# The group norms of the opening moved behind the masks of levels 1 and 2, and fewer warm matmuls in the turn

## The reference, cut to what matters

```python
# delta-rule attention: batch 4, heads 8, sequence 768, head size 48
k_n = k / (norm(k) + 1e-6)
for t in range(768):
    y[t] = q[t] @ state
    state += beta[t] * outer(k_n[t], v[t] - state^T k_n[t])
# gated layer: 3072 tokens, 384 -> 1536 -> 384
x = (sigmoid(x @ w_gate) * (x @ w_val)) @ w_out
# routed layer: 8 experts, one per token, 384 -> 1024 -> 384
e = argmax(cosine(x, expert_emb) / tau);  gate = softmax probability of e
out = gate * (relu(x @ w1[e]) @ w2[e])
```

## Time and profile before

| | |
|---|---|
| median of 3 executions | 1217.78 us (1216.74 to 1219.96) |
| the profiled execution | 1220.51 us, its span 1218.8 us |
| TensorE busy | 1191.5 us, 98% of the span |
| VectorE, ScalarE, GpSimd busy | 57%, 41%, 48% |
| mean granted clock of TensorE | 0.995 of 2.4 GHz |
| chain that ended last | TensorE 91%, VectorE 3%, transfers 2% |

### The profile page before, as it was taken

How to read it: one execution, slowest core, us unless ns; L and a number is a source line. 1 busy time by engine, 2 the same in 40 slices (tenths; PEclk the granted TensorE clock), 3 DMA queues, 4 the chain that set the end, 5 groups by cost and what they waited for, 6 DMA issues and landing times.

```text
span 1218.8 us, 29243 instructions
## 1 busy us (share of the span) xinstructions
PE 1191.5 (98%) x11548; PEld 1090.4 (89%) x11548; DVE 696.1 (57%) x1539; ACT 498.6 (41%) x1143; POOL 579.4 (48%) x590
## 2 busy tenths in 40 slices
PE   6899999999999999999999999999999999999997
PEld 2669999999999999999999999999968899989996
DVE  5665566766566666656666665653564945555000
ACT  5644433343443334344433434442214444444443
POOL 5773334333343434324343432322337877777764
PEclk9999999999999999999999999999989999999999
DMA  7451011001111111110111111002016431443110
GB/s 225 113 170 29 24 40 30 30 30 30 36 29 36 30 30 29 30 43 24 34 30 32 27 30 36 8 22 88 31 34 234 140 127 57 156 165 107 45 39 1
DMA packets 48247, 74.76 MB, mean 61 GB/s; under 512 B 7797, under 2 KB 36789, under 8 KB 48116
## 3 DMA queue, kind: packets, MB, share of 16 engines
q1 hardware_dynamic: 41396, 61.82, 15.7%
q0 software_dynamic: 6720, 11.07, 3.0%
HBM read 61.59 MB, written 12.65 MB: 61 GB/s over the span
## 4 chain that ended last, share of the span: by engine, by line
PE 91%; DVE 3%; DMA 2%; ACT 1%; issue 1%; POOL 1%; SPq 1%; POOLq 0%; DVEq 0%
PE ps L1330 27%; PE ps L1345 13%; PE ps L1569 6%; PE ps L1585 6%; PE ps L1195 3%; PE ps L1574 3%; PE ps L1290 3%; PE ps L1589 3%; PE ps L1299 3%; PE ps L1220 3%; PE ps L1212 3%; PE ps L1223 2%; PE ps L1350 2%; PE ps L1599 2%; PE ps L1297 2%; PE ps L1267 2%
## 5 line engine op out<-in xcount | busy, mean ns | idle before, releaser
L440 POOL TENSOR_TENSOR gl<-sg,gh 128x256 fp32r<-128x256 f32 x144 | 108.2, 751 | 392.1 <-ACT gh L994 392.0
L1330 PE MATMUL ps<-xh,wgh 128*128 128x256 f32 x864 | 263.7, 305 | 0.0
L1330 PE MATMUL ps<-xl,wgh 128*128 128x256 f32 x864 | 243.4, 282 | 0.0
L1330 PE MATMUL ps<-xh,wgl 128*128 128x256 f32 x864 | 242.7, 281 | 0.0
L664 DVE TENSOR_TENSOR MP<-ps,mE 128x512 f16<-128x512 f32 x126 | 87.1, 691 | 153.2 <-PE ps L1212 150.3
L1330 PEld LDWEIGHTS ps<-xh,wgh 128*128 128x128 f32 x864 | 163.7, 189 | 7.9 <-issue 7.0
L1330 PEld LDWEIGHTS ps<-xl,wgh 128*128 128x128 f32 x864 | 164.2, 190 | 0.0
L1330 PEld LDWEIGHTS ps<-xh,wgl 128*128 128x128 f32 x864 | 163.6, 189 | 0.0
L990 ACT ACTIVATE sg<-ps 128x256 f32<-128x256 f32 x144 | 55.4, 385 | 262.0 <-PE ps L1330 262.0
L947 ACT CAST Xs<-ps 128x512 f16<-128x512 f32 x126 | 73.6, 584 | 142.1 <-PE ps L1220 142.1
L1345 PE MATMUL ps<-woh,gh 128*128 128x392 f32 x288 | 108.9, 378 | 1.2 <-POOL gl L440 1.2
(11 more groups left out here) (215 smaller groups left out, 2637.2 us busy)
## 6 DMA issues: line engine op xcount, KB each, us to landing
W<-w_dram SPq DMA_DIRECT2D x16, 1536.0 KB, 10.4
betaT<-betaT_dram SPq DMA_DIRECT2D x48, 128.0 KB, 3.0
kin<-kv_dram SPq DMA_DIRECT2D x24, 192.0 KB, 2.6
kqT<-qT_dram SPq DMA_DIRECT2D x48, 96.0 KB, 2.6
vin<-kv_dram SPq DMA_DIRECT2D x24, 192.0 KB, 2.4
x_dram<-x2r SPq DMA_DIRECT2D x24, 192.0 KB, 2.0
woT<-woT_dram SPq DMA_DIRECT2D x1, 2304.0 KB, 9.0
stage<-w_gate_dram SPq DMA_DIRECT2D x6, 384.0 KB, 9.4
```

The lines of the kernel that those rows point to most:

```text
L440: pool.tensor_tensor(gl[n % 2][:, :], gp[n % 2][:, :], gh[n % 2][:, :].bitcast(F32), ALU.subtract).then_inc(gl_ok, 1)
L1330: mm = pe.matmul(ps[n % 2][:, kind * TB:(kind + 1) * TB], w[:, kind, a, cs], v[m % 2][:, a, :], start=(a == 0 and x == 0), stop=(a == KT - ...
```

## The change

VectorE's opening runs `norm_a` behind the masks of level 1 and `norm_b`, `norm_c` behind those of level 2. GpSimd's opening runs the second weight piece of a step behind `scaled_keys` instead of behind `keys`, so that nothing but the first piece stands ahead of its wait for the norms. `split_piece(5)` moves into the last body step, and the second batch of warm matmuls in the turn has 20 instead of 36.

```diff
@@ GpSimd, opening(s)
             keys(s + 1)
             if s == 0:
                 tables()
-            weight_low(6 * s + 1)
             inverse_low(s, 0)
             inverse_low(s, 1)
             scaled_keys(s + 1)
-            for n in range(6 * s + 2, 6 * s + 6):
+            for n in range(6 * s + 1, 6 * s + 6):
                 weight_low(n)
@@ VectorE, body(s)
             if settled(s) is not None:
                 gate_c(settled(s))
+            if s == NS - 1:
+                split_piece(5)
@@ VectorE, opening(s)
-            norm_a(s + 1)
-            norm_b(s + 1)
-            norm_c(s + 1)
             for l in range(1, LEVELS):
                 for hf in range(2):
                     half_mask(s, l, hf)
+                if l == 1:
+                    norm_a(s + 1)
+                if l == 2:
+                    norm_b(s + 1)
+                    norm_c(s + 1)
                 if l == 2 and cg is not None:
                     state_update(cg)
@@ VectorE, behind the gates
-        for c in range(5, WC // PIECE):
+        for c in range(6, WC // PIECE):
             split_piece(c)
@@ TensorE, turn
         pe.wait_ge(tab_ok, 1)
-        warm(36)
+        warm(20)
         wait(pe, pay_ok, NM)
```

## The result

The changed kernel takes **1225.3 us** (1224.83 to 1228.27, 6 runs) where the kernel before, timed beside it, takes 1218.09 (1216.74 to 1220.18, 6 runs): ratio 1.0057, 95% interval 1.0045 to 1.0069; the medians differ by +7.2 us. Forecast was +10.1 over the median.

The account below looks back on a forecast made before the run. TensorE, busy in 98% of the span, was the bound, with waits on VectorE's norms (opening) and warm matmuls (turn). Opening +10.0, clock +3.0, turn -2.6 gave +10.4: 1230.9 from the profiled 1220.5, less 2.7, 1228.2 us; range 1217 to 1233.

Parts of the forecast that it names:

- the prediction's own signs: Profile after: step 1 CT near 6 us, L886 near 3, mask 1 at 51.7 or later; CT under 2 refutes.
- The norms, on VectorE: Opening: mask 1 to mask 3 becomes 4.86; step 0 nets 0, step 1 +0.1, step 2 -0.98.
- The -0.9 of the norms alone: Opening steps 0 to 2: what moving the norms brings without GpSimd's lateness, -0.9 us.
- GpSimd's queue, step 0: Opening: late rn puts keys at 26.96, 5.1 later; the weight string ends at 46.8 instead of 42.56.
- Loads and ScalarE: Opening: later loads put the copy of W at 45.0 instead of 42.45; ScalarE's wait in step 3 is free.
- The wait this adds: Opening: VectorE's CT waits out GpSimd's whole string, +4.24 in step 1, +7.3 in step 2; opening +10.0.
- Rival (a): Opening: VectorE gets the port between two GpSimd operations; total +2.4, 1220.2 us; chance 0.16.
- Rival (c): Opening: all three clock falls at full price, +9.7 instead of +3, about 1234.5 us; chance 0.12.
- Clock: Opening: TensorE clock falls behind new idles of about 5, 2.7 and 3.3 us cost +3, 2 for the first.
- Turn: Turn: 16 fewer warm matmuls bring the gates' transpose forward, -2.6 us; `split_piece(5)` alone 0.
- Sum: Whole kernel: +10.0 + 3.0 - 2.6 = +10.4, forecast 1228.2 us.

Follow-up runs that it names:

- The held-back kernel: Changed kernel, with GpSimd waiting in steps 1 and 2 for XTs before its first two weight pieces, taken ahead of keys: 1217.76 us, ratio 0.999.
- turning the order in the expert phase: Kernel before with the change's turn edits, and GpSimd's indirect write moved behind its two hidden_low instead of ahead: 1215.75 us, ratio 0.9976.
- the profiled one with the warm matmuls: Changed kernel plus 11 warm matmuls (6 and 5) in TensorE's waits at the start of step 3: 1222.32 us, ratio 1.0037.
- that of the norms alone: Kernel before with only VectorE's norms moved, GpSimd's order and the turn as before: 1225.72 us, ratio 1.0049.
- the turn alone: Kernel before with only `split_piece(5)` moved and 16 fewer warm matmuls: 1216.58 us, ratio 0.9979.

## Why the prediction was right, and which step was wrong

The direction and the cause held: rn is late, and GpSimd's string meets VectorE's CT and XTs. The size did not: +10.4 was summed up and +7.2 came, and that the time lies inside the range is owed to the width that the rivals gave it. By the prediction's own signs its main mechanism failed: a CT under 2 us was to make it wrong, and CT took 1.90; L886 (L889 after) took 1.19 and not 3, mask 1 of step 1 stood at 49.8 (with the offset) and not at 51.7, and the first inverse of body 3 came 4.1 later and not 10 to 13.

- *The norms, on VectorE*: 4.86 from mask 1 to mask 3 was forecast, it is 5.01, with mask 3 as TensorE's new wait. Right. The -0.9 of the norms alone was not: it rests on the 4.59 of step 2, which was a clock fall. With 3.49 there, step 2 nets +0.1 like step 1. The held-back kernel agrees: without most of GpSimd's lateness the cut is worth nothing that the times show.
- *GpSimd's queue, step 0* and *Loads and ScalarE*: right within 0.5 in step 1 (keys at 26.96, copy of W at 45.03). In step 3 ScalarE's wait for the last piece was not free: it reached VectorE ahead of L889. Moving the second piece was counted as part of the cost; alone it measures 0.
- *The wait this adds*: **the step that failed is "VectorE does not get in between two queued GpSimd operations".** It was read from one row pair, in which an indirect transfer's issue stood ahead of the pair. CT takes 1.90, not 6.3; halving the pieces and turning the order in the expert phase both show the boundary. The Trainium skill (Trainium Architecture — The Big Picture, What this means for kernel authors) calls the port that the two engines share an exclusive lock, not a split of bandwidth. The rows agree, with CT at 1.90 behind one piece and the next piece at 2.25 behind CT, and they show when the lock passes: at the end of one instruction, so that the two engines take turns.
- Rival (a) had exactly this, at +3.2, +3.9 and +5 for steps 1, 2 and 3; 2.66, 4.0 and 4.8 were found (the last two against a step 2 without a clock fall). It had a chance of 0.16, against a forecast at 0.55 with +10.0. It left out the clock: its 1220.2 with some 2.5 for the fall, and 0.9 less for the turn, comes to 1223.6. (Rival (c) was mis-summed by 0.4: 1228.2 + 6.7 is 1234.9.)
- *Clock*: +3 was forecast, 2 of it for step 1. Some 2.5 came, but in step 3 in the trace of after, behind idles of 1.04 and 0.89; step 1, with an idle of 1.87 rather than 5, kept 2.4 GHz. The prediction set an idle of 2.26 that passed as the mark and overlooked the fall in step 2 of its own trace, behind an idle of 1.25. Where a fall comes varies even between kernels whose step 1 is nearly the same: in the profiled one with the warm matmuls the clock was 0.72 from 44 to 50 and from 54 to 60, in that of the norms alone 0.54 from 44 to 50.
- *Turn*: -2.6 holds where the clock has fallen ahead of it, as in both traces here; where it hasn't, the gates end the saving at some -1.9. The times of the turn alone (-1.7 by the medians, -2.6 by the ratio) can't tell the two apart.
- *Sum*: +10.0 + 3.0 - 2.6 against about +6 (the +8.6 of the opening less the clock), +2.5 and -1.7, all by the medians. The first term was too large by 4, by the failed step; the two others were each off by under 1.

## What to carry to other kernels

When an operation moves on one engine, follow its signal to the in-order queue that waits for it, and then look at what that queue meets on the shared port: the cost here was neither on the engine that was edited nor in the operations moved. Price such a meeting at no more than the rest of one instruction of the other engine for each operation that meets it (an indirect transfer's issue was the exception here), and make long background instructions wait until the operations on the chain are through, but check what they meet instead. An idle of TensorE is worth its length plus, at times, a clock fall: here 2 to 3 us behind 1.9 of idle, and 11 filler matmuls took that part back. Read the granted clock of the trace of before in the same way: a stretch that looks slow may be a fall and not the code.

## What the runs showed of the hardware that was not expected

- The port changed hands at the end of single instructions: beside one queue of 1.8 us pieces, CT took 1.90, XTs 1.91 and CT 1.77 in a row, and the piece behind CT took 2.25 instead of 1.81. With instructions of half the size they took 1.53, 1.10 and 1.13, and the string took longer, 10.24 for ten.
- A very small operation waits as well: one of 128x8, 0.17 by itself, waited 1.25.
- One case is different: 3.6 to 3.9 us for a 0.95 us operation that begins during the issue of an indirect transfer with two instructions right behind it.
- Two idles of about 1 us in step 3 were followed by 6 us at 1.2 GHz, while an idle of 1.87 in step 1 of the same execution was not.
